# Attention, two gated products and a maximum of three in float32: scores a block ahead, and operands prepared at another place

## The chip, the cores and the metric

One core of one Trainium2 chip. The time is device microseconds of one launch. Before: 1257.44 us, median of three runs (1254.42 to 1262.59). The engines are TensorE (PE), VectorE (DVE), ScalarE (ACT), GpSimd (POOL) and SyncE (SP); each works its own instructions in order and waits on semaphores that the others raise. DMAs are started by SP and POOL.

## The reference

```python
# attention: 4 x 8 heads, 768 tokens, 64 wide; chunks of 32 tokens see 8 memory keys, 16 to the left, 8 to the right
scores = scale * (q_c @ k_full.T); scores -= max(scores)
a = exp(scores); a = a / (sum(a) + 1e-09)
x = a @ v_full                                   # then x: 3072 tokens x 512
h = x @ w_in                                     # 512 -> 2048
y = (h * cos(h)) @ w_out                         # 2048 -> 512
z = maximum(maximum(y @ w1, y @ w2), y @ w3)     # 512 -> 768
out = z @ w_out2                                 # 768 -> 512
```

Everything is float32.

## The kernel before

**Numbers.** A matmul on the fast float32 form rounds its operands, so each operand is held in two parts: `high`, a rounded copy that ACT makes, and `low`, the remainder that DVE (for w_in POOL) makes from raw and high. A product is three matmuls (`three`, L544 to L548): high x high, high x low, low x high. Of the four large products, the last three are done by seven products of half-size blocks in place of eight; for that, DVE or POOL first forms four sums of each raw operand (`sums_g`, `sums_w2`, `sums_h` and others, seven 256-column pieces per operand), then ACT rounds the seven pieces (1792 columns) and DVE makes the low part.

**First stage (L650).** Eight blocks `t` of 384 tokens. A block is 16 half tiles `f` of h (`hidden`, 12 matmuls of 384 columns each); two half tiles are a tile, which ACT evacuates (`evacuate`, two passes), DVE reduces to a turn (`turn`), ACT takes through Sin and Square (`cosine`) and DVE multiplies (`gated`); POOL stores it to DRAM. One tile later the same for the next, with two pairs of banks. Between the half tiles PE does the attention of the next block (`attend`, L615) for its three groups of 128 tokens: `scores_of`, after which DVE takes maximum and difference (`shift`) into the one probability buffer and ACT the exponential of all three (`exps`, L780); `turn_probs`, copied by ACT (`copy_probs`); `values`, scaled by DVE (`normalise`); `turn_out`, rounded by ACT and DVE into x (`x_high`, `x_low`). In blocks after the first the scores, the transposes, the weighted values and x's transposes have one bank each. q/k and v of the first three groups have a buffer each, later groups share one of each kind, and SP loads a group when PE is done with the one before. w_in is loaded by POOL through three buffers, converted in block 0.

**Second product (L673).** 48 units `n`, eight to a block `b` of 512 tokens; a unit is 42 matmuls of 256 columns. g's operand is loaded by SP (two raw buffers, `load_g`), summed by DVE, rounded by ACT (`high_g`), and its rest made by DVE (`low_g`, L1096), two units ahead, into three slots. At the last unit of a block ACT copies two of the seven sums out (y11 and p5, L938 and L943) and DVE adds the others; PE opens a bank again when it has been read. SP stores y at the next unit, ahead of that unit's load of g; the loads of y come in the same queue.

**Third stage (L764).** 36 units of the three products with maximum (384 columns; nine to a block, three weights times three), then 12 of the last product (256 columns, two to a group of 512 tokens). In each step ACT copies three sums out (`snap`), DVE adds and compares (`c22`, `c11`, `c12`, `c21`, `largest`). In the first block of this stage the weights are converted on the way: POOL loads w2's unit and forms sums (`load_w2`, `sums_w2`), ACT and DVE do high and low at the end of step `n` for unit `n + 1`. For the last product z comes back from DRAM: SP loads (`load_h`), DVE sums, ACT and DVE round, at the end of the step that the list `HIGH_H` (L67) names for each of the 18 operands `r`; two steps of PE wait for three of them. The last stores of z and the loads share SP's queue.

The waits that order all this are written out by hand; three of them at the heart of it:

```python
pe.wait_ge(shifted, n)                 # scores_of: the bank is read
dve.wait_ge(pt_done, n - NSUB + 1)     # shift: the probabilities of the block before are turned
act.wait_ge(unit_done, n - 2)          # high_g: the slot is free
```

## Time and profile before

| | |
|---|---|
| runs | 1262.59, 1254.42, 1257.44 us |
| profiled execution | 1261.36 us, span 1259.6 us |
| mean granted TensorE clock | 0.919 |
| PE busy | 1037.5 us, 82% of the span |
| DVE busy | 686.4 us, 54% |
| ACT busy | 512.6 us, 41% |
| POOL busy | 156.4 us, 12% |
| HBM traffic | 107 GB/s over the span |

The busy time of an engine is the sum of its instructions; the clock is the share of full speed that PE was granted. The span is cut, by what PE works on, at 36.9 us (first half tile of h), 93.0 (block 1), 447.5 (block 7), 481.0 (first unit of the second product), 818.6 (first step of the third stage) and 922.4 (second block of it); the last product begins near 1119 us.

### The profile page before, as it was taken

The page shows a single profiled execution, that of the slowest core. Times are in us where ns is not written, and L with a number is a line of the kernel's source. Part 1 is how long each engine was busy: PE and PEld are TensorE (multiplying, and loading weights), DVE is VectorE, ACT ScalarE, POOL GpSimd, SP SyncE. Part 2 cuts the span into 40 slices and gives each one's busy share as a digit, 9 for nine tenths or more (in the row PEclk, how much of TensorE's full clock was granted, in tenths as well). Part 3 has the DMA queues.
Part 4 walks back from the last instruction along what each step waited for, and adds up shares of the span by engine and source line. Part 5 has one row for each costly group of instructions (what it writes and reads, how often), then busy time and mean ns, then how long its engine had stood idle before and what let it go on. Part 6 is the DMA issues. An engine that isn't in the chain of part 4 may idle for free.

```text
span 1259.6 us, 18304 instructions
## 1 busy us (share of the span) xinstructions
PE 1037.5 (82%) x7564; PEld 997.0 (79%) x7564; DVE 686.4 (54%) x926; ACT 512.6 (41%) x641; POOL 156.4 (12%) x199
## 2 busy tenths in 40 slices
PE   5797877888788799688778686877699999996887
PEld 4687777777777799688778686777699999986876
DVE  4444545354535467656666565844464646675462
ACT  1575646556555686322323232323232323433231
POOL 3540101010101112100100000044110001100000
PEclk6998989899989999989898897989899999998888
DMA  9654445353534335232332324142111211233331
GB/s 200 170 150 125 139 115 145 106 160 106 153 109 135 92 112 165 84 117 87 113 103 84 101 84 151 37 133 74 59 76 51 75 45 49 92 118 101 117 101 67
DMA packets 73587, 135.41 MB, mean 108 GB/s; under 512 B 5920, under 2 KB 39712, under 8 KB 73504
## 3 DMA queue, kind: packets, MB, share of 16 engines
q1 hardware_dynamic: 61856, 94.39, 25.9%
q0 software_dynamic: 11648, 39.85, 9.4%
q8 instruction: 60, 0.98, 0.4%
q14 instruction: 23, 0.19, 0.1%
HBM read 87.03 MB, written 47.19 MB: 107 GB/s over the span
## 4 chain that ended last, share of the span: by engine, by line
PE 41%; DVE 25%; ACT 15%; DMA 11%; issue 6%; SPq 2%; DVEq 0%; ACTq 0%
PE ps L546 12%; PE ps L548 12%; PE ps L547 12%; DVE units L1099 7%; ACT units L831 5%; DMA work<-qk_in 4%; DMA work<-v_in 3%; DMA work<-g_dram 2%; PE ps L587 2%; PE ps L562 2%; DVE work L1088 2%; DVE work L1086 2%; DVE work L1090 2%; ACT work L808 1%; DVE units L1143 1%
## 5 line engine op out<-in xcount | busy, mean ns | idle before, releaser
L546 PE MATMUL ps<-units 128*128 128x384 f32 (+1 forms) x1940 | 644.1, 332 | 124.9 <-DVE units L1099 44.7
L547 PE MATMUL ps<-units 128*128 128x384 f32 (+1 forms) x1940 | 628.6, 324 | 0.0
L548 PE MATMUL ps<-units 128*128 128x384 f32 (+1 forms) x1940 | 627.9, 324 | 0.0
L546 PEld LDWEIGHTS ps<-units 128*128 128x128 f32 x1940 | 394.1, 203 | 144.7 <-issue 83.4
L547 PEld LDWEIGHTS ps<-units 128*128 128x128 f32 x1940 | 394.1, 203 | 0.0
L548 PEld LDWEIGHTS ps<-units 128*128 128x128 f32 x1940 | 393.0, 203 | 0.0
L831 ACT CAST units<-work 128x1792 fp32r<-128x1792 f32 x48 | 80.9, 1686 | 233.8 <-DVE work L1090 233.8
L965 ACT COPY work<-ps 128x384 f32<-128x384 f32 (+1 forms) x144 | 63.6, 453 | 221.3 <-PE ps L548 221.3
L1058 DVE SCALAR_TENSOR_TENSOR work<-work 128x768 f32<-128x768 f32 x64 | 62.7, 980 | 148.1 <-ACT work L808 148.1
L1099 DVE TENSOR_TENSOR units<-work,units 128x1792 fp32r<-128x1792 f32 x48 | 97.1, 2023 | 70.1 <-ACT units L831 70.1
L805 ACT ACTIVATE work<-ps 128x768 f32<-128x768 f32 x64 | 51.8, 809 | 130.9 <-PE ps L548 130.2
L441 POOL DMA_DIRECT2D g_dram<-work x64 | 46.5, 727 | 361.8 <-DVE work L1063 355.0
L1278 DVE TENSOR_TENSOR work<-work,ps 128x384 f32<-128x384 f32 (+1 forms) x48 | 24.9, 519 | 115.5 <-PE ps L548 115.5
L1063 DVE SCALAR_TENSOR_TENSOR work<-work 128x768 f32<-128x768 f32 x64 | 61.9, 968 | 42.0 <-ACT work L815 41.9
L808 ACT ACTIVATE work<-ps,rounder 128x768 f32<-128x768 f32 x64 | 57.3, 896 | 1.6 <-DVE work L1063 1.6
L815 ACT ACTIVATE work<-work 128x768 f32<-128x768 f32 x64 | 54.1, 845 | 2.0
L813 ACT ACTIVATE work<-work 128x768 f32<-128x768 f32 x64 | 54.0, 844 | 0.1
L562 PE MATMUL ps<-work 128*32 128x128 f32 x704 | 26.9, 298 | 32.8 <-DMA work<-qk_in 18.2
L562 PEld LDWEIGHTS ps<-work 128*32 128x32 f32 x704 | 20.4, 118 | 39.0 <-issue 38.9
L1143 DVE TENSOR_TENSOR units<-work,units 128x1792 fp32r<-128x1792 f32 x18 | 36.1, 2024 | 17.7 <-ACT units L871 17.5
L465 POOL DMA_DIRECT2D work<-w_in x12 | 6.5, 549 | 313.6 <-DVE units L1105 294.7
L1299 DVE TENSOR_TENSOR work<-work,ps 128x384 f32<-128x384 f32 (+1 forms) x48 | 24.9, 519 | 35.8 <-PE ps L548 35.7
(100 smaller groups left out, 806.5 us busy)
## 6 DMA issues: line engine op xcount, KB each, us to landing
g_dram<-work POOLq DMA_DIRECT2D x64, 384.0 KB, 3.6
work<-g_dram SPq DMA_DIRECT2D x48, 512.0 KB, 3.8
work<-qk_in SPq DMA_DIRECT2D x44, 384.0 KB, 5.3
work<-w_in POOLq DMA_DIRECT2D x50, 256.0 KB, 3.2
work<-v_in SPq DMA_DIRECT2D x44, 256.0 KB, 4.1
...
```

Source lines behind the costliest of these rows:

```text
L546: pe.matmul(o, wh, mh, start=start, stop=False, skip_group_check=onto)
L547: pe.matmul(o, wh, ml, start=False, stop=False, skip_group_check=onto)
L548: return pe.matmul(o, wl, mh, start=False, stop=stop, skip_group_check=onto)
L562: mm = pe.matmul(scores(n)[chunk, a, :, :], q[:, a, KC + CH * c:KC + CH * c + CH], two_parts(q, a, c, KC + SUB), start=True, stop=True)
L808: act.activation(ang(i), hidden_banks(i), ACT.Identity, scale=1.0 / (2 * PI), bias=rounder[:, :])\
L813: act.activation(ang(i), ang(i), ACT.Sin, scale=BELOW_PI).then_inc(sin_done, 1)
L815: act.activation(ang(i), ang(i), ACT.Square, scale=ROOT_TWO).then_inc(square_done, 1)
L831: act.copy(operand(9 + n % 3)[:, 0, :, :], graw[n % 2]).then_inc(g_high, 1)
L965: act.copy(tile[:, 0:span_of(n)], bank).then_inc(copied, 1)
L1058: dve.scalar_tensor_tensor(out=ang(i), in0=ang(i), scalar=ROUND, in1=hid(i), op0=ALU.subtract, op1=ALU.subtract).then_inc(r_done, 1)
L1063: dve.scalar_tensor_tensor(out=hid(i), in0=ang(i), scalar=1.0, in1=hid(i), op0=ALU.subtract, op1=ALU.mult).then_inc(g_done, 1)
L1099: dve.tensor_tensor(g[:, 1, :, :], graw[n % 2], g[:, 0, :, :].bitcast(F32), ALU.subtract).then_inc(g_ready, 1)
```

## The change

In the first stage the order of the attention's steps among the half tiles changes. Three buffers of q/k serve the groups up to the ninth and three of v those up to the sixth, where they served the first three, and v's loads are whole rows. In block `t` (from 1 on) PE turns the probabilities of block `t + 1` and does the scores of block `t + 2`, whose exponential ACT takes at half tile 14; block 0 does the scores of blocks 1 and 2. w_in gets 16 raw buffers in space that later operands use, and SP loads it. `high_g` and `low_g` work in two parts, four pieces and three, of which the first needs two of the four sums. ACT copies y11 before it rounds g. The first load of y moves from unit 40 to unit 24 in SP's queue, and the preparations of y and of w2 in the second product move. In the third stage weights and h are rounded at the head of a step, w2 for unit `n + 2`; a part of h's sums goes to POOL; `HIGH_H` names earlier steps for eight operands, and SP loads h by that list. The diff, cut:

```diff
-HIGH_H = (32, 33, 34, 35, 36, 37, 38, 38, 39, 40, 40, 41, 42, 42, 43, 44, 44, 45)
+HIGH_H = (32, 33, 34, 35, 36, 37, 37, 38, 38, 39, 40, 40, 41, 42, 42, 43, 44, 44)
...
+        raw_rows = [plain(f"raw_wi{i}", at, 512 * n) for i, (at, n) in
+                    enumerate(((2560, 2), (UCOLS + 2560, 2), (2 * UCOLS + 2048, 3), (3 * UCOLS + 2048, 3),
+                               (4 * UCOLS, 6)))]
+        raw_wi = [rows[:, 512 * i:512 * (i + 1)] for rows, n in zip(raw_rows, (2, 2, 3, 3, 6)) for i in range(n)]
...
+        def sums_h(eng, r):
+            done, base = h_sums[r % 3], 4 * (r // 3)
+            t = raw_d[r % 3]
+            eng.wait_ge(h_landed[r % 3], 16 * (r // 3) + 16)
...
             load_qk(0)
+            load_qk(1)
             load_v(0)
-            load_qk(1)
+            load_wi(0)
             load_qk(2)
             load_v(1)
             load_v(2)
-            load_qk(NSUB)
-            load_v(NSUB)
-            for n in range(NSUB + 1, SUBS, NSUB):
+            for f in range(1, 6):
+                load_wi(f)
+            for n in range(NSUB, 2 * NSUB):
                 load_qk(n)
-                load_qk(n + 1)
-                if n + 2 < SUBS:
-                    load_qk(n + 2)
+                load_wi(2 * n)
+                load_wi(2 * n + 1)
+            for n in range(NSUB, 2 * NSUB):
                 load_v(n)
-                load_v(n + 1)
-                if n + 2 < SUBS:
-                    load_v(n + 2)
+                if n < 2 * NSUB - 1:
+                    load_wi(2 * n + 6)
+                    load_wi(2 * n + 7)
+            for n in range(2 * NSUB, 3 * NSUB):
+                load_qk(n)
+            load_v(2 * NSUB)
+            load_qk(3 * NSUB)
+            for n in range(2 * NSUB + 1, SUBS):
+                load_v(n)
+                if n + 3 < SUBS:
+                    load_qk(n + 3)
             for n in range(4):
...
-                if n == UNITS1 - FPAIRS:
+                if n == 3 * FPAIRS:
                     load_y(0)
...
-                if m % TAUS == 0:
-                    for r in range(NPAIR * (m // TAUS + 2), min(NPAIR * (m // TAUS + 3), HUNITS)):
+                for r in range(2 * NPAIR, HUNITS):
+                    if max(HIGH_H[r - NPAIR], UNITS_A + 1) == UNITS_A + 1 + m:
                         load_h(r)
...
-            load_wi(0)
...
-            pool.wait_ge(v_landed[0], 32)
-            load_wi(1)
-            load_wi(2)
...
-                if f + 3 < NF:
-                    pool.wait_ge(wi_ready, f + 1)
-                    load_wi(f + 3)
...
+            for r in range(HUNITS):
+                if r < 2 * NPAIR or r % 2 == 0:
+                    sums_h(pool, r)
...
+            def attend_first(f):
+                n = NSUB
+                if f == 0:
+                    scores_of(n)
+                elif f == 2:
+                    scores_of(n + 1)
+                elif f == 4:
+                    scores_of(n + 2)
+                elif f == 7:
+                    turn_probs(n)
+                elif f == 9:
+                    values(n)
+                    turn_probs(n + 1)
+                elif f == 10:
+                    turn_out(n)
+                    turn_probs(n + 2)
+                elif f == 11:
+                    values(n + 1)
+                    scores_of(n + NSUB)
+                elif f == 12:
+                    turn_out(n + 1)
+                    scores_of(n + NSUB + 1)
+                elif f == 13:
+                    values(n + 2)
+                elif f == 14:
+                    turn_out(n + 2)
+                    scores_of(n + NSUB + 2)
...
                 n = NSUB * (t + 1)
-                if t < NBLK - 1:
...
+                later = t < NBLK - 2
+                if f == 1:
+                    turn_probs(n)
+                elif f == 3:
+                    values(n)
+                elif f == 4:
+                    turn_probs(n + 1)
+                    turn_out(n)
+                elif f == 6:
+                    turn_probs(n + 2)
+                    if later:
                         scores_of(n + NSUB)
+                elif f == 7:
+                    values(n + 1)
+                elif f == 8:
+                    turn_out(n + 1)
+                elif f == 9 and later:
+                    scores_of(n + NSUB + 1)
+                elif f == 11:
+                    values(n + 2)
+                elif f == 12:
+                    turn_out(n + 2)
+                    if later:
+                        scores_of(n + NSUB + 2)
...
+            scores_of(0)
+            scores_of(1)
+            turn_probs(0)
+            values(0)
+            scores_of(2)
...
-                    attend(t, f)
+                    if t == 0:
+                        attend_first(f)
+                    elif t < NBLK - 1:
+                        attend(t, f)
...
+            def high_g(n, part):
+                act.wait_ge(g_sums, 4 * n + 2 * part + 2)
+                if part == 0:
+                    if n < 3:
+                        act.wait_ge(h_done, TILES - FPAIRS + (2, 4, 5)[n])
+                    else:
+                        act.wait_ge(unit_done, n - 2)
+                q = slice(0, 4) if part == 0 else slice(4, 7)
+                act.copy(operand(9 + n % 3)[:, 0, q, :], graw[n % 2][:, q, :]).then_inc(g_high, 1)
...
+                if u == UNITS - 1:
+                    act.wait_ge(w2_ready, u)
                 raw = raw_late if u >= 3 and u % 2 else raw_w
                 act.copy(operand(s)[:, 0, :, :], raw).then_inc(w2_high, 1)
 
@@ -861,7 +937,7 @@
                 act.copy(operand(SLOT_V[v])[:, 0, :, :], raw_d[v]).then_inc(v2_high, 1)
 
             def high_h(r):
-                act.wait_ge(h_sums, 4 * r + 4)
+                act.wait_ge(h_sums[r % 3], 4 * (r // 3) + 4)
                 if r < 6:
                     act.wait_ge(p_done[4], UNITS_A - UNITS + 3 + r + 1)
                 elif r < 9:
...
+                    if first and f == 5:
+                        exps(0, NSUB, n + NSUB)
                     if f % 2:
                         i = FPAIRS * t + f // 2
                         evacuate(i)
+                        if first and f == 7:
+                            copy_probs(n)
+                        elif first and f == 9:
+                            copy_probs(n + 1)
+                        elif first and f == 15:
+                            exps(0, NSUB, n + 2 * NSUB)
+                        elif f == 1 and not last and not first:
+                            copy_probs(n)
...
+                    elif not last:
+                        if f == 4:
+                            copy_probs(n + 1)
+                            x_high(n)
+                        elif f == 6:
+                            copy_probs(n + 2)
+                        elif f == 8:
+                            x_high(n + 1)
+                        elif f == 12:
+                            x_high(n + 2)
+                        elif f == 14 and t < NBLK - 2:
+                            exps(0, NSUB, n + 2 * NSUB)
+                    if 1 <= t < 6 and f == 10:
                         high_w1(t - 1)
...
-                if n and n + 2 < UNITS1:
-                    high_g(n + 2)
                 if i == FPAIRS - 1:
                     act.wait_ge(whole_done[1], b + 1)
                     if b:
                         act.wait_ge(y_stored[(b - 1) % 2], y_total(b - 1))
                     act.copy(y11, ps[:, BANK1[1], :]).then_inc(y1_copied, 1)
+                if n and n + 2 < UNITS1:
+                    high_g(n + 2, 0)
+                    high_g(n + 2, 1)
+                if i == FPAIRS - 1:
...
                 if n == 41:
                     high_y(0, 1)
+                    high_y(0, 5)
                 elif n == 42:
-                    high_y(0, 5)
-                elif n == 43:
                     high_y(0, 2)
                     high_y(0, 6)
+                elif n == 43:
+                    high_y(0, 3)
+                    high_y(0, 7)
                 elif n == 44:
-                    high_y(0, 3)
+                    high_y(0, 4)
                 elif n == 45:
-                    high_y(0, 7)
-                    high_y(0, 4)
-                elif n == 46:
                     high_w2(1)
+                elif n == 47:
+                    high_w2(2)
...
+                if 1 <= n <= 6:
+                    high_w2(n + 2)
+                if UNITS_A - 7 <= n < UNITS_A - 4:
+                    high_v2(n - UNITS_A + 7)
+                rows = [r for r in range(HUNITS) if HIGH_H[r] == n]
+                if rows:
+                    high_h(rows[0])
                 if n < UNITS_ALL:
                     snap(n, 1, bank_b(n), snap1, c11_done, n, s1_copied)
                     if n < UNITS_A and u == UNITS - 1 and blk < NBLK2 - 1:
                         high_y(blk + 1, 1)
+                    if rows[1:]:
+                        high_h(rows[1])
...
-                if 1 <= n <= 7:
-                    high_w2(n + 1)
-                if UNITS_A - 7 <= n < UNITS_A - 4:
-                    high_v2(n - UNITS_A + 7)
-                for r in range(HUNITS):
-                    if HIGH_H[r] == n:
-                        high_h(r)
...
+            def low_g(n, part):
+                dve.wait_ge(g_high, 2 * n + part + 1)
+                q = slice(0, 4) if part == 0 else slice(4, 7)
                 g = operand(9 + n % 3)
-                dve.tensor_tensor(g[:, 1, :, :], graw[n % 2], g[:, 0, :, :].bitcast(F32), ALU.subtract).then_inc(g_ready, 1)
+                low = dve.tensor_tensor(g[:, 1, q, :], graw[n % 2][:, q, :], g[:, 0, q, :].bitcast(F32), ALU.subtract)
+                if part:
+                    low.then_inc(g_ready, 1)
...
+                        elif f == 8:
+                            sums(0, NSUB, NSUB + 1)
+                    elif f == 2 and not last:
+                        sums(0, NSUB, NSUB + t + 1)
...
+                    if first:
+                        if f == 9:
                             normalise(n)
                         elif f == 10:
+                            x_low(n)
+                        elif f == 11:
                             normalise(n + 1)
+                            shift(n + NSUB)
+                        elif f == 12:
+                            shift(n + NSUB + 1)
+                            x_low(n + 1)
+                        elif f == 13:
+                            normalise(n + 2)
+                        elif f == 14:
+                            shift(n + NSUB + 2)
+                            x_low(n + 2)
+                    elif not last:
+                        if f == 3:
+                            normalise(n)
+                        elif f == 4:
                             x_low(n)
+                        elif f == 6 and t < NBLK - 2:
+                            shift(n + NSUB)
+                        elif f == 7:
+                            normalise(n + 1)
+                        elif f == 8:
+                            x_low(n + 1)
+                        elif f == 9 and t < NBLK - 2:
+                            shift(n + NSUB + 1)
                         elif f == 11:
                             normalise(n + 2)
                         elif f == 12:
-                            x_low(n + 1)
-                        elif f == 13:
+                            if t < NBLK - 2:
+                                shift(n + NSUB + 2)
                             x_low(n + 2)
-                    if 1 <= t < 6 and f == 12:
+                    if 1 <= t < 6 and f == 5:
                         sums_w1(t - 1)
-                    if 1 <= t < 6 and f == 15:
+                    if 1 <= t < 6 and f == 14:
                         low_w1(t - 1)
...
                     low_w2(0)
-                if n == 41:
-                    y_sum(0, 0)
-                elif n == 42:
+                if n in (30, 31):
+                    y_sum(0, n - 30)
+                elif n == 41:
                     y_low(0, 1)
                     y_low(0, 5)
-                    y_sum(0, 1)
+                elif n == 42:
                     y_sum(0, 2)
-                elif n == 43:
                     y_low(0, 2)
                     y_low(0, 6)
+                elif n == 43:
                     y_sum(0, 3)
+                    y_low(0, 3)
+                    y_low(0, 7)
                 elif n == 44:
-                    y_low(0, 3)
+                    y_low(0, 4)
                 elif n == 45:
-                    y_low(0, 7)
-                    y_low(0, 4)
-                elif n == 46:
                     low_w2(1)
+                elif n == 47:
+                    low_w2(2)
...
+                rows = [r for r in range(HUNITS) if HIGH_H[r] == n]
+                if 1 <= n <= 6:
+                    low_w2(n + 2)
+                if UNITS_A - 7 <= n < UNITS_A - 4:
+                    v2_low(n - UNITS_A + 7)
+                if rows:
+                    low_h(rows[0])
                 if n:
                     c22(before)
                     if before < UNITS_A and before % NB2:
                         largest(before)
                 if renew:
                     y_low(blk + 1, 1)
+                if rows[1:]:
+                    low_h(rows[1])
                 if n < UNITS_ALL:
                     c11(n)
+                for r in range(2 * NPAIR, HUNITS):
+                    if r % 2 and HIGH_H[r] == n + 1:
+                        sums_h(dve, r)
...
```

## Rows read from the trace of the kernel before

**Rows 1.** windows: us, busy of PE, PEld, DVE, ACT, POOL, clock, DMA share, GB/s

```profile
36.90:93.00 56.10, 45.49 (x409) 42.13 (x410) 24.58 (x29) 36.91 (x51) 29.92 (x33) 0.97 0.61 167
93.00:447.50 354.50, 286.38 (x2417) 265.38 (x2417) 170.04 (x217) 203.32 (x251) 41.80 (x58) 0.92 0.45 128
447.50:481.00 33.50, 33.50 (x193) 33.50 (x194) 25.17 (x33) 28.98 (x35) 6.89 (x10) 1.00 0.34 117
481.00:818.60 337.60, 269.73 (x2018) 264.72 (x2017) 218.09 (x293) 100.43 (x76) 15.14 (x19) 0.91 0.32 100
560.00:584.00 24.00, 24.00 (x202) 24.00 (x201) 15.38 (x21) 7.91 (x5) 0.00 (x0) 1.00 0.33 103
818.60:922.40 103.80, 77.27 (x385) 74.90 (x384) 46.61 (x55) 29.61 (x44) 38.53 (x46) 0.90 0.24 81
922.40:1107.00 184.60, 184.01 (x1056) 182.80 (x1056) 106.34 (x148) 57.75 (x104) 10.18 (x12) 1.00 0.19 71
1107.00:1259.60 152.60, 119.36 (x828) 116.19 (x828) 80.53 (x128) 47.04 (x72) 0.00 (x0) 0.88 0.30 99
```

**Rows 2.** waits of PE: line, what it waited for, us in total, times, longest us

```profile
PE ps L546 <- DVE units L1099: 44.7, 15, 8.5
PE ps L573 <- ACT work L784: 28.1, 7, 4.0
PE ps L546 <- DVE units L1105: 26.0, 7, 4.8
PE ps L546 <- DVE units L1143: 24.7, 5, 5.0
PE ps L546 <- ACT work L938: 20.0, 5, 4.2
PE ps L587 <- DMA work<-v_in: 19.6, 9, 3.4
...
PE ps L546 <- ACT work L965: 4.9, 8, 1.1
```

**Rows 3.** timeline of PE around 606 us: start, us, line, shapes, idle before it

```profile
606.64 0.58 PE L546 MATMUL ps<-units 128*128 128x256 f32 x1 [4.83 <-DVE units L1099]
...
612.57 0.40 PE L546 MATMUL ps<-units 128*128 128x256 f32 x1
...
613.04 0.28 PE L546 MATMUL ps<-units 128*128 128x256 f32 x1
```

**Rows 4.** timeline of POOL, one load of w2 and its first sum

```profile
860.35 1.08 POOL L465 DMA_DIRECT2D work<-w_in  x2 [3.49 <-DVE units L1105]
864.04 0.73 POOL L474 TENSOR_TENSOR work<-work 128x256 f32<-128x256 f32 x1 [2.61 <-DMA work<-w_in]
```

**Rows 5.** timeline of PE, one group of scores

```profile
226.06 1.08 PE L562 MATMUL ps<-work 128*32 128x128 f32 x32 [1.96 <-DMA work<-qk_in]
```

**Rows 6.** timeline of ACT ahead of an Exp

```profile
172.12 0.81 ACT L805 ACTIVATE work<-ps 128x768 f32<-128x768 f32 x1 [6.15 <-PE ps L548]
...
174.49 0.84 ACT L815 ACTIVATE work<-work 128x768 f32<-128x768 f32 x1
175.35 1.28 ACT L784 ACT_TABLE_LOAD   x1
176.65 1.48 ACT L784 ACTIVATE work<-work 128x1536 f32<-128x1536 f32 x1
```

**Rows 7.** timeline of DVE, the gating of the same tile

```profile
175.37 0.96 DVE L1063 SCALAR_TENSOR_TENSOR work<-work 128x768 f32<-128x768 f32 x1 [0.58 <-ACT work L815]
```

**Rows 8.** timeline of DVE at a boundary of the second product

```profile
594.93 0.68 DVE L1246 TENSOR_TENSOR work<-work,ps 128x512 f32<-128x512 f32 x1
601.01 0.42 DVE L1084 TENSOR_TENSOR work<-work 128x256 f32<-128x256 f32 x1 [5.40 <-DMA work<-g_dram]
...
604.56 2.02 DVE L1099 TENSOR_TENSOR units<-work,units 128x1792 fp32r<-128x1792 f32 x1 [1.75 <-ACT units L831]
```

**Rows 9.** timeline of SP, first loads of h behind the last store

```profile
1129.26 4.96 SPq L352 DMA_DIRECT2D work<-h_dram  x2
```

221 lines of the change are left out of this document (94 added, 127 removed).

## Prediction

> **What bounds the kernel now.** First I cut the span where its stages change and read the busy times by window [rows 1]. TensorE (PE) is the engine with the most work, and two windows show what it does when nothing stops it: the last block of the first stage (447.50 to 481.00, no attention) is 33.5 us for 193 matmul records, all busy at clock 1.00, and 922.40 to 1107.00 is 184.0 us busy of 184.6. So a long dense stretch keeps the full clock here. Everything else is a loss against that: the six attention blocks take 354.5 us (59.1 each) at clock 0.92, the 48 units of the second product take 337.6 us at 0.91, the first nine steps of the third stage 103.8 us, the end 152.6 us at 0.88.
>
> Second, who PE waited for [rows 2]. The order is by total, but the count and the longest matter more: 4.0 us seven times for the Exp, some 4.9 us five times for h (L1143), up to 4.8 us seven times for w2 (L1105), 4 us five times for the y11 copy (L938), and L1099 with 44.7 us over 15. These are regular stalls of a schedule, not of a saturated engine.
>
> Third, what a stall costs beyond itself [rows 3]. After 4.83 us of idleness a 256-column matmul lasts 0.41 us in the place of 0.28; 28 of them stand 0.21 apart where full speed has 0.12, which is 2.7 us more: the lower of the two levels, 1.2 and 2.4 GHz. A stall of 4 to 5 us costs about 2.7 beyond its length; where the wait is 2 to 3 us I count half of that, as an estimate between nothing and 2.7.
>
> **Front (before the first hidden matmul, 36.9 us).** The loads of scores 1 go ahead of the values of 0, scores 2 go behind values 0, and w_in's loads leave POOL for SP. The first score groups wait on loads, the rest on a chain of ACT and DVE steps. Bounds: no gain (the same bytes must land) to 8 us (the load of one group taken out of the way twice, at the 3.7 us of the w2 load [rows 4]). I take 4, nearer the chain, which stays.
>
> **Block 0.** It loses the waits for q/k and v, for there are three buffers, but takes three more score groups of 1.08 us [rows 5] and both exponentials, and ACT also converts w_in. One exponential is a table load of 1.28 and 1.48 us of work [rows 6], and another table load leads back to Sin, so two cost ACT 8.1 us in a block where it is already busy 36.9 of 56.1 [rows 1]. I take no change, between 5 us gained and 5 lost.
>
> **Blocks 1 to 6.** Pure work is 33.5 + 3 score and 3 value groups of 1.08 + six groups of transposes at an estimated 0.4 (four 128-column matmuls, between 4 times 0.06 by the 256-column spacing and 1.08) = 42.4 us. What goes: the Exp wait, since it ran at half tile 14 of the block before; the score wait for the shift; and q/k and v loads, whose buffers are now freed three or four half tiles (2.09 us each) and their attention groups ahead, 8 us and more, against 6.2 us now (two half tiles and the wait of 1.96 [rows 5]). The v loads also go row by row in one piece. If that cover failed, v alone would bring back what [rows 2] shows for it, 19.6 us in all.
> What is late next is `turn_out`. It stands one half tile behind its `values`, and DVE does `normalise` only after `gated`, which waits for ACT. From the end of an odd half tile ACT takes 3.23 us for evacuation, Sin and Square [rows 6], `gated` 0.96 [rows 7], and `normalise` is like the 128x512 add of 0.68 [rows 8]: ready after 4.9 us. PE gets there after 1.08 + 2.09 = 3.2 us (3.6 with transposes between). That is 1.7 us, twice a block. At the first one ACT is behind: the Exp at half tile 14 makes 3.23 + 1.28 + 1.48 = 6.0 us for a slot of 4.2, the Sin reload adds 1.28, and each tile gives back about 1 us, so 1.3 us are left: 2.7 us. Together 6.1 us a block, and 1.5 us for a low stretch behind the first. A block is then 50.0 us, and block 6, without scores ahead, 46.8: 296.8 for six, 58 less. Bounds 35 (the waits double) to 72 (half of them hidden).
> The table load is the one place where a rule would move the sum. The row shows Square of 0.84 us beginning at 174.49, the load at 175.35 and Exp at 176.65 [rows 6]: a switch costs 1.3 us. The Trainium skill (ScalarE: Activation LUTs, What ACT_TABLE_LOAD costs) counts a drain of about 1.38 us beside the load, 2.66 us in all, for each switch. By it ACT would be 2.8 us later after each Exp and the sum about 17 us worse; the trace has no such drain, so I do not take it.
>
> **Second product, 48 units.** A unit is 42 matmuls; 202 in 24.00 us [rows 1] make it 4.99 us, 240 for 48, so 98 us are lost now. (a) The y11 copy stands before the rounding of g, where ACT is free once the first product has been summed; five waits of 4 us and their low stretches go. What is queued behind it is the rounding, 0.6 us later, with two units of slack. (b) In two parts the chain of one g is two sums 0.9, high part 4/7 of the 1.75 that DVE waits for it = 1.0, low parts 4/7 and 3/7 of 2.02 = 1.15 and 0.87, some 4.0 us, where now sums, rounding and remainder follow one another for 5.6 us (601.01 to 604.56 + 2.02) [rows 8]; 5.6 is over the unit's 4.99, 4.0 is not. (c) The store of y ahead of the next g load stays. From the last add of y (594.93) to the sums of g (601.01) are 6.1 us, and that add will begin 7.3 us after the start of its unit (two adds end at 2.9, the low parts at 4.9, then five adds 0.6 apart); the g is ready 17.4 us after it, PE wants it after 15.0: 2.4 us left of 4.8. (d) `load_y(0)` is moved, not removed: the longest wait on L1099, 8.5 against 4.8, puts its price at 3.7 us, now at unit 24. Left over: 4 x 2.4 + 6.1 = 15.7, about 5 for low stretches, 1 for w1 at the start and 3 for the y operands at the end: 265 us, 73 less (55 to 85).
>
> **Third stage, first nine steps.** 385 matmuls at 33.5/193 us are 66.8 us, so 37 are lost. Unit n + 1 was rounded behind step n; now n + 2 is, at the head, so the rounding itself is covered by a step of 42 x 0.174 = 7.3 us. Next is POOL: load to sums 3.7 us, four sums of 0.8 us [rows 4], 7.0 to 8 us a unit, about PE's pace. And ACT and DVE now wait at the head for those sums, with the copies of the step's sums queued behind them, for which PE's sixth and fourth products wait. w2 unit 2 is some 2.5 us late and unit 3, which may load only when the last unit is done, some 5 us; with the drift of POOL and one low stretch 13 us stay: 24 less (10 to 32).
>
> **End.** The waits on L1143 are 24.7 us, with about 2.7 each for the clock 38, and 5 on L965 [rows 2]: 43 lost. The sums of h on POOL, and rounding two steps earlier, cover 6.2 + 1.7 + 2 us of chain. But r = 6 is due at step 37, where its load leaves SP only behind the last store of the group before, 2.1 us into that step (1129.26) [rows 9]. It lands some 4.3 us later (3.7 for the smaller w2 load [rows 4]), four sums are 3.2, rounding 1.75: 11.4 us into the step, and the copy that PE's sixth product needs at 5.3 is queued behind it. That is 6 us, 2.7 for the clock and 2 of small waits: 11 stay, 32 less (20 to 40).
>
> **Sum.** 4 + 0 + 58 + 73 + 24 + 32 = 191 us. The profiled execution took 1261.4 us (span 1259.6 and 1.8 around it), 3.9 above the median of 1257.4; 1261.4 - 191 = 1070, and 1068 set between that and the same against the median.
>
> **Rivals.** *ACT becomes the bound of the blocks*: its copies, both table loads and the wait of `x_high` for `turn_out` add up, so a block keeps 59 us. For it: ACT has no gap between evacuation and Square [rows 6]; against: busy 203 of 354.5 us [rows 1]. 1068 + 58 = 1126, chance 0.14, in which I count that the scores are not really ahead because one probability buffer holds them.
> *The heads block*: ACT waits at the head of steps and stalls the copies, so fill and end win nothing: 1068 + 56 = 1124, chance 0.08.
> *g stays late*: only the y11 copy is won, 34 of 73 us: 1107, chance 0.08.
> *A table switch costs twice its row*: with ACT's queue full, the load of 1.28 is preceded by as long a pause. Two in each of six blocks are 2.6 us, all on the first wait: 16 us, 1084, chance 0.05. The rule of the Trainium skill named above (ScalarE: Activation LUTs, What ACT_TABLE_LOAD costs) says this.
> *Less is left*: `turn_out` finds its input because PE's pace gives ACT time: 6 x 7.6 us less, 1022; chance 0.13. That block 0 showed small waits at clock 0.97 speaks for it.
> *Slower*: the clock in the attention blocks. Three short waits a block could hold it at the low level throughout. A block's 42 us double, less the 6 of waits: 36 each, 216 for six, 1284. It decides from more than 5.3 of the six blocks at the low level. Against: the blocks now have longer waits and still 0.92 and 0.97 [rows 1]. Chance 0.02.
>
> **Numbers.** My forecast has 0.50. The range 1030 to 1128 takes the unknown terms' bounds, most of the rivals and half of *less is left*. A change of 1%, 13 us, is about what can be told from none. Faster by more than 1%: 0.96; within it 0.02 (several rivals at once); slower 0.02.
>
> **What would show it.** Blocks of 50 us with waits on the vector engine's L1045 line before `turn_out` and none on v, q/k or Exp; no wait on the y11 copy; one wait of 2 to 3 us each eight units; steps of 7.3 us in the fill but for the first two; one wait of 6 us at step 37. Wrong if blocks stay near 59 us, or if ACT's copies are what PE waits for in the third stage.

## The result, and the profile after

The kernel after takes 1103.65 us, the median of four runs (1098.38 to 1105.35), beside 1255.93 us of the kernel before, four runs: ratio 0.8775, interval 0.8726 to 0.8824. The profiled execution has a span of 1101.0 us, 158.6 less than before, at a mean granted clock of 0.957. The forecast was 1068 us, with a range of 1030 to 1128: the direction and the range held, and the point lies 36 us too low.

The same cuts as before, by what PE works on, give this table of windows (us, then busy of PE, PEld, DVE, ACT, POOL, then clock, DMA share, GB/s; PEld is TensorE's loading of weights). First the kernel before, cut on its very first matmuls, for the third stage up to the last product and for the last product, which [rows 1] does not have as one line:

```profile
818.40:1118.40 300.00, 272.07 (x1502) 268.39 (x1501) 162.10 (x214) 92.41 (x154) 48.71 (x58) 0.97 0.21 75
1118.40:1259.60 141.20, 108.78 (x769) 105.69 (x768) 71.58 (x117) 42.00 (x63) 0.00 (x0) 0.87 0.30 99
```

Then the kernel after: front, block 0, blocks 1 to 6, second product, third stage, last product. Block 7, left out here, takes 33.5 us as before.

```profile
0.00:33.20 33.20, 20.41 (x233) 16.31 (x233) 14.89 (x26) 7.96 (x14) 9.76 (x17) 0.63 0.99 215
33.20:99.60 66.40, 53.04 (x505) 47.70 (x506) 29.50 (x36) 36.45 (x51) 24.92 (x23) 0.90 0.73 175
99.60:409.20 309.60, 269.28 (x2351) 248.93 (x2351) 164.10 (x210) 204.58 (x251) 41.41 (x57) 0.97 0.48 137
...
442.70:720.90 278.20, 253.12 (x2018) 250.46 (x2017) 222.40 (x340) 105.37 (x123) 14.28 (x19) 0.96 0.39 123
720.90:994.80 273.90, 266.19 (x1502) 262.72 (x1502) 157.63 (x201) 93.00 (x155) 68.73 (x79) 0.99 0.24 83
994.80:1101.00 106.20, 95.51 (x770) 94.89 (x768) 58.17 (x81) 38.92 (x62) 31.34 (x28) 0.97 0.37 127
```

| part | before | after | change | predicted |
|---|---|---|---|---|
| front | 36.9 | 33.2 | -3.7 | -4 |
| block 0 | 56.1 | 66.4 | +10.3 | 0 (-5 to +5) |
| blocks 1 to 6 | 354.5 | 309.6 | -44.9 | -58 |
| second product | 337.5 | 278.2 | -59.3 | -73 |
| third stage, up to the last product | 300.0 | 273.9 | -26.1 | -24 |
| last product | 141.2 | 106.2 | -35.0 | -32 |

Part of block 0's 66.4 us is this one execution: in the seven other kernels that keep its order of steps (experiments 4 and 6 to 11) the block takes 62.6 to 64.4 us.

Busy time of the other engines barely tells of it (DVE 672.2 us for 686.4, ACT 515.6 for 512.6, POOL 197.7 for 156.4): what went are waits, and with them the low level of TensorE's clock. The waits of PE after, against [rows 2] (line, what it waited for, total, times, longest):

```profile
PE ps L629 <- DVE o_natural L1144: 47.0, 21, 6.9
PE ps L579 <- DVE units L1199: 22.5, 8, 8.2
PE ps L579 <- ACT work L1062: 13.7, 7, 6.4
PE ps L620 <- ACT prob_turned L862: 9.5, 10, 2.6
```

The Exp (28.1 us before), v (19.6), w2's rest (26.0), h's rest (24.7) and the copy of y11 (20.0) are gone from the list. What is new at its head is `turn_out` waiting for `normalise` (L1144), as the prediction said. A block has one wait of 3.1 us and two of 1.6 (timeline of PE, the waits in brackets):

```profile
116.57 0.66 PE L629 MATMUL ps<-ident,o_natural 128*128 128x128 f32 x4 [3.10 <-DVE o_natural L1144]
...
131.62 0.66 PE L629 MATMUL ps<-ident,o_natural 128*128 128x128 f32 x4 [1.59 <-DVE o_natural L1144]
...
144.68 0.66 PE L629 MATMUL ps<-ident,o_natural 128*128 128x128 f32 x4 [1.59 <-DVE o_natural L1144]
...
168.77 0.99 PE L629 MATMUL ps<-ident,o_natural 128*128 128x128 f32 x4 [3.10 <-DVE o_natural L1144]
```

From 116.57 to 168.77 is the period of a block: 52.2 us, before 59.1, predicted 50.0. DVE's timeline ahead of the first of them shows why the wait is there at all:

```profile
111.94 1.75 DVE L1129 TENSOR_REDUCE ssum<-work 128x24 f32<-128x1536 f32 x1
...
114.15 0.90 DVE L1157 SCALAR_TENSOR_TENSOR work<-work 128x768 f32<-128x768 f32 x1
114.97 0.95 DVE L1162 SCALAR_TENSOR_TENSOR work<-work 128x768 f32<-128x768 f32 x1
115.83 0.68 DVE L1144 TENSOR_TENSOR o_natural<-ps,sinv 128x512 f32<-128x512 f32 x1
```

The normalisation (L1144) needs 0.68 us and stands behind the turn (L1157) and the gating (L1162) of a tile of h, which need what ACT makes of that tile. In front of those, at the first of the three, the sum over the probabilities (L1129) takes another 1.75 us. Little of that sum is on the path: ACT's last pass for this gating (L887) ends at 114.56, and the gating begins at 114.97.

### The profile page after: what moved, and what is told of

It reads as the page before. It is cut to its first block, busy times and chain, and to the rows that moved or that the text cites. A ratio compares the mean times of both kernels' runs of the same rounds, so it can differ in the third digit from the quotient of the medians.

```text
span 1101.0 us, 18400 instructions
## 1 busy us (share of the span) xinstructions
PE 991.0 (90%) x7564; PEld 954.5 (87%) x7564; DVE 672.2 (61%) x926; ACT 515.6 (47%) x689; POOL 197.7 (18%) x231
## 4 chain that ended last, share of the span: by engine, by line
PE 49%; DVE 16%; ACT 16%; DMA 10%; issue 5%; POOL 3%; SPq 1%; DVEq 0%; ACTq 0%
PE ps L579 15%; PE ps L581 15%; PE ps L580 15%; DVE units L1199 5%; DMA work<-g_dram 3%; ACT work L885 3%; ACT work L887 2%; ACT work L880 2%; ACT work L877 2%; DVE work L1162 2%; PE ps L595 2%; ACT units L905 2%; PE ps L629 2%; DMA work<-w_in 1%; DMA work<-h_dram 1%
## 5 line engine op out<-in xcount | busy, mean ns | idle before, releaser
L579 PE MATMUL ps<-units 128*128 128x384 f32 (+1 forms) x1940 | 622.2, 321 | 41.6 <-DVE units L1199 22.5
L580 PE MATMUL ps<-units 128*128 128x384 f32 (+1 forms) x1940 | 612.0, 315 | 0.0
L581 PE MATMUL ps<-units 128*128 128x384 f32 (+1 forms) x1940 | 611.9, 315 | 0.0
L579 PEld LDWEIGHTS ps<-units 128*128 128x128 f32 x1940 | 378.0, 195 | 57.0 <-DVE units L1199 24.5
L580 PEld LDWEIGHTS ps<-units 128*128 128x128 f32 x1940 | 377.9, 195 | 0.0
L581 PEld LDWEIGHTS ps<-units 128*128 128x128 f32 x1940 | 377.4, 195 | 0.0
L905 ACT CAST units<-work 128x1024 fp32r<-128x1024 f32 x96 | 85.7, 938 | 154.8 <-DVE work L1185 141.7
L1062 ACT COPY work<-ps 128x384 f32<-128x384 f32 (+1 forms) x144 | 63.0, 453 | 136.9 <-PE ps L581 136.8
L1157 DVE SCALAR_TENSOR_TENSOR work<-work 128x768 f32<-128x768 f32 x64 | 61.9, 967 | 99.1 <-ACT work L880 99.1
L1199 DVE TENSOR_TENSOR units<-work,units 128x1024 fp32r<-128x1024 f32 x96 | 102.1, 1105 | 10.2 <-ACT units L905 10.2
L1162 DVE SCALAR_TENSOR_TENSOR work<-work 128x768 f32<-128x768 f32 x64 | 61.3, 957 | 47.8 <-ACT work L887 47.7
L629 PE MATMUL ps<-ident,o_natural 128*128 128x128 f32 x96 | 18.7, 329 | 47.0 <-DVE o_natural L1144 47.0
L629 PEld LDWEIGHTS ps<-ident,o_natural 128*128 128x128 f32 x96 | 12.0, 161 | 54.1 <-DVE o_natural L1144 53.3
L1234 DVE TENSOR_TENSOR units<-work,units 128x1792 fp32r<-128x1792 f32 x18 | 39.6, 2201 | 31.1 <-ACT units L947 31.1
L1400 DVE TENSOR_TENSOR work<-work,ps 128x384 f32<-128x384 f32 (+1 forms) x48 | 24.8, 516 | 55.3 <-PE ps L581 55.3
L887 ACT ACTIVATE work<-work 128x768 f32<-128x768 f32 x64 | 54.1, 846 | 2.0
L1183 DVE TENSOR_TENSOR work<-work 128x256 f32<-128x256 f32 x48 | 20.1, 420 | 35.7 <-DMA work<-g_dram 35.7
```

The costliest lines, as they stand in the source:

```text
L579: pe.matmul(o, wh, mh, start=start, stop=False, skip_group_check=onto)
L580: pe.matmul(o, wh, ml, start=False, stop=False, skip_group_check=onto)
L581: return pe.matmul(o, wl, mh, start=False, stop=stop, skip_group_check=onto)
L887: act.activation(ang(i), ang(i), ACT.Square, scale=ROOT_TWO).then_inc(square_done, 1)
L905: act.copy(operand(9 + n % 3)[:, 0, q, :], graw[n % 2][:, q, :]).then_inc(g_high, 1)
L1062: act.copy(tile[:, 0:span_of(n)], bank).then_inc(copied, 1)
```

## The experiments

"Before" and "after" are the two kernels. Where the stages of an experiment matter, they are cut at the same first matmuls as above. One fact is needed to read them: kernels with the same first stage begin their second product anywhere from 437.2 to 442.8 us (after itself 442.75, the HIGH_H experiment 437.22), so an effect in block 0 is read from its own waits and length and not from the total.

### 1. The copy of y11 ahead of the rounding of g, alone, on the kernel before

```diff
-                if n and n + 2 < UNITS1:
-                    high_g(n + 2)
                 if i == FPAIRS - 1:
                     ...
                     act.copy(y11, ps[:, BANK1[1], :]).then_inc(y1_copied, 1)
+                if n and n + 2 < UNITS1:
+                    high_g(n + 2)
```

> The kernel before, with one edit: at the last unit of a block of the second product ACT copies y11 ahead of the rounding of g. Theory: the copy is behind the rounding in ACT's queue and nothing else holds it, so the five waits of 4 us on it (20.0 us in all) and the low clock stretches behind them (5 times 1.6 us) go: 28 us less for the second product, 337.5 to 310 us, 1228 us in all. Rival: g is late anyway (its chain is 5.6 us a unit), so the waits turn up on the low part of g at the same units or the next, and less than 10 us is won.

Measured: 1245.72 us, ratio 0.9893 (0.9857 to 0.9930), 13 us less. The second product goes from 337.5 to 327.5 us. The waits on the copy are gone, but PE then waits for the additions to y, and for g as before:

```profile
527.48 0.38 PE L546 MATMUL ps<-units 128*128 128x256 f32 x1 [1.34 <-DVE work L1229]
...
544.89 0.58 PE L546 MATMUL ps<-units 128*128 128x256 f32 x1 [5.10 <-DVE units L1100]
```

So the 20 us of [rows 2] on L938, with their low stretches, were worth 10: the rest moved to the next link.

### 2. g rounded in two parts, alone, on the kernel before

```diff
-                act.copy(operand(9 + n % 3)[:, 0, :, :], graw[n % 2]).then_inc(g_high, 1)
+                for part, q in ((0, slice(0, 4)), (1, slice(4, 7))):
+                    act.wait_ge(g_sums, 4 * n + 2 * part + 2)
+                    ...
+                    act.copy(operand(9 + n % 3)[:, 0, q, :], graw[n % 2][:, q, :]).then_inc(g_high, 1)
```

(and so for the remainder, `low_g` on DVE.)

> The kernel before, with one edit: rounding and remainder of g in two parts of four and three pieces, the order of the queues as before. Theory: the chain of one g falls from 5.6 to 4.0 us and the waits on g at units 3 to 7 (7.8 us) go; the five at the block's third unit lose 1.5 us each, but the y11 copy still waits behind both parts: 16 us less, 1240 us in all. Rival: the copy of y11 comes 0.1 us later and the added instructions eat the rest: no change within 5 us.

Measured: 1201.03 us, ratio 0.9548 (0.9512 to 0.9584), 57.6 us less. The second product takes 282.3 us, 55 of the 59 that the whole change wins there. The line for the waits on g, 44.7 us in 15 of [rows 2], becomes

```profile
PE ps L546 <- DVE units L1102: 22.6, 8, 7.1
```

and of the five waits on the y11 copy one of 1.90 us is left, though the copy still stands behind the rounding. That is the point: ACT was late with the copy because it stood waiting for the sums of a late g. ACT's timeline in the kernel before shows it, with the copy (L938) at the end:

```profile
581.45 1.69 ACT L831 CAST units<-work 128x1792 fp32r<-128x1792 f32 x1 [3.81 <-DVE work L1090]
586.94 1.68 ACT L831 CAST units<-work 128x1792 fp32r<-128x1792 f32 x1 [3.81 <-DVE work L1090]
588.53 0.58 ACT L938 COPY work<-ps 128x512 f32<-128x512 f32 x1
```

The roundings are 5.49 us apart, and PE takes 5.04 us for a unit without a wait, so g falls behind by 0.45 us a unit. With two parts they follow every 4.00 us (535.16, 539.16, 543.16 in this experiment) until ACT has to wait for PE.

### 3. Both, on the kernel before

The edits of 1 and 2 together.

> The kernel before, with both edits of the second product: y11 copied first, g in two parts; the first load of y at unit 40 as before. Theory: the two add up to 28 + 16 and a little more, since after the copy the adds of y end sooner: 48 us less, 1208 us in all, with one wait of 2 to 3 us left in each block and 6 to 8 us at unit 42. Rival: they cover the same waits and together give no more than the larger one alone, 28 us.

Measured: 1196.33 us, ratio 0.9513 (0.9465 to 0.9561), 62 us less; second product 278.6 us, which is the 278.2 of after. The two edits are the whole gain of that stage, and the split carries it; alone 13 and 58, together 62: in part they remove the same stall.

### 4. w2 rounded one unit ahead at the end of a step again, on the kernel after

```diff
-                if 1 <= n <= 6:
-                    high_w2(n + 2)
 ...
+                if 1 <= n <= 7:
+                    high_w2(n + 1)
```

(the same for `low_w2` on DVE.)

> The changed kernel with one part taken back: w2 rounded at the end of step n for unit n + 1, unit 2 at the end of step 1, as before. Theory: the part was worth what the third stage lost of its waits (26 us between the two traces, of which h has next to nothing), so this kernel is 22 to 28 us slower than the changed one: 1129 us, with the seven waits of 2.7 to 4.8 us on w2's low part back. Rival: the earlier conversion of unit 1 and of y in the second product, which stays, already carries most of it: under 10 us slower.

Measured: 1128.09 us, ratio 0.8961 (0.8922 to 0.9001), 24.4 us more than after. The third stage takes 301.6 us, as before the change (300.0), and the seven old waits are back:

```profile
PE ps L579 <- DVE units L1205: 25.5, 7, 4.6
```

The gain of the third stage is this one move, in which the lead of a unit and the place at the head of a step were not tried apart. The time rises by less than the 27.7 us of the stage, since this execution reached its second product 3.9 us earlier than after.

### 5. `normalise` ahead of turn and gating, on the kernel after

```diff
+                    if not last and f in ((9, 11, 13) if first else (3, 7, 11)):
+                        normalise(n + ((9, 11, 13) if first else (3, 7, 11)).index(f))
                     if f % 2:
                         ...
-                        if f == 3:
-                            normalise(n)
```

(and so for the other five places.)

> The changed kernel with one edit: at the half tiles where DVE scales the weighted values it does so ahead of the turn and the gating, not behind them. Theory: the waits of 3.1, 1.6 and 1.6 us a block ahead of the transposes of the output (47.0 us over all blocks) are this order alone, since the values are there 1.1 us after the half tile and DVE is idle then; they go with the low clock stretch behind the first, 1.7 us a block: 55 us less, 1049 us. Rival: ACT, which rounds the turned output behind its own queue, is the bound, and the wait moves to x or to the next transposes: under 20 us less.

Measured: 1054.31 us, ratio 0.8398 (0.8354 to 0.8441), 49 us less than after. One wait of 1.6 us a block is left, and the block's period is 45.5 us:

```profile
195.94 0.66 PE L629 MATMUL ps<-ident,o_natural 128*128 128x128 f32 x4 [1.60 <-DVE o_natural L1144]
241.48 0.66 PE L629 MATMUL ps<-ident,o_natural 128*128 128x128 f32 x4 [1.60 <-DVE o_natural L1144]
```

A window over nearly four of these periods has clock 1.00:

```profile
147.90:329.00 181.10, 172.72 (x1621) 160.82 (x1622) 112.22 (x147) 134.99 (x165) 28.33 (x39) 1.00 0.59 162
```

6.3 us of waits a block in after, 1.6 here; 6.7 us of period less. The other 2 us are the low stretch behind the wait of 3.1. It also gives the work of PE in a block: 45.5 - 1.6 = 43.9 us, a wait of 0.3 on `copy_probs` included, where the prediction had 42.4.

Blocks 1 to 6 give 38 of the 49 us. Block 0 gives 9, or 6 against the 63.3 us that it takes in most other executions of this order:

```profile
30.89:87.98 57.09, 50.48 (x504) 45.84 (x505) 29.93 (x36) 36.35 (x50) 25.02 (x23) 0.94 0.83 205
```

That is 1.1 us more than the 56.0 of the kernel before, and the wait at the first `turn_out` is 1.82 us, for 6.91. Yet the stores of g still take 8.1 us to land here, and ACT still waits for one of them before it evacuates:

```profile
65.41 0.81 ACT L877 ACTIVATE work<-ps 128x768 f32<-128x768 f32 x1 [3.63 <-DMA g_dram<-work]
```

Experiments 6 and 11 ask about those stores; this one shows that most of block 0's loss is the order on DVE.

### 6. q/k of groups 7 and 8 loaded behind v of group 6, on the kernel after

```diff
-            for n in range(2 * NSUB, 3 * NSUB):
-                load_qk(n)
+            load_qk(2 * NSUB)
             load_v(2 * NSUB)
+            load_qk(2 * NSUB + 1)
+            load_qk(2 * NSUB + 2)
```

> The changed kernel with one edit in SP's queue: the loads of q/k for groups 7 and 8 stand behind that of v for group 6, so they leave some 15 us later in block 0. Theory: block 0 is 10 us longer than before because the 16 DMA engines are full until 72 us and the stores of the gated tiles take 8.1 us in the place of 3.6, for which ACT waits before it evacuates; with less in flight the stores land in 4 to 5 us, the wait of 6.9 us shrinks by 3 to 4 us and the kernel is 4 us faster, 1100 us. Rival: ACT's own work in block 0 (w_in, two Exp) makes that wait, and nothing changes within 1.5 us in block 0.

Measured: 1102.70 us, ratio 0.8779 (0.8736 to 0.8822), 1 us less than after, which is nothing that these runs can tell. The first wait of block 0 at `turn_out` falls all the same, from 6.91 to 3.48 us; in the five kernels with this part of the queue unchanged (experiments 4, 7, 8, 9 and 10) it is 5.2 to 6.2. The wait got shorter and the time did not: block 0 takes 63.1 us. Experiment 11 goes on from there.

### 7. The load of g ahead of the store of y, on the kernel after

```diff
+                if n >= 2 and n + 2 < UNITS1:
+                    load_g(n + 2)
                 if n % FPAIRS == 0 and n:
                     store_y(n // FPAIRS - 1)
                 if n == 3 * FPAIRS:
                     load_y(0)
-                if n >= 2 and n + 2 < UNITS1:
-                    load_g(n + 2)
```

> The changed kernel with one edit in SP's queue: in the second product the load of g goes ahead of the store of y (and of the load of y) of the same unit. Theory: the wait left at the third unit of each block (3.8, 2.4, 8.2, 2.8 and 2.3 us) is the load queued behind the store, which waits for the last add of y; all five go with their low stretches of 1.8 us: 26 us less, 1077 us. Rival: SP's wait on g's buffer then delays the store, and with it the next block's sums or the load of y, or g is late through DVE: under 8 us less.

Measured: 1073.76 us, ratio 0.8564 (0.8505 to 0.8623), 30 us less than after. The second product takes 252.2 us (278.2); it also began 3.8 us earlier, where nothing was edited. In after SP's queue at unit 24 reads, and DVE's sums begin 10 us late:

```profile
581.28 3.30 SPq L343 DMA_DIRECT2D y_dram<-work  x6
584.74 1.23 SPq L357 DMA_DIRECT2D work<-y_dram  x2
586.07 16.37 SPq L334 DMA_DIRECT2D work<-g_dram  x4
```

```profile
593.91 0.42 DVE L1183 TENSOR_TENSOR work<-work 128x256 f32<-128x256 f32 x1 [10.26 <-DMA work<-g_dram]
```

The line of waits on g, 22.5 us in 8, becomes

```profile
PE ps L579 <- DVE units L1199: 4.7, 5, 2.2
```

### 8. The list HIGH_H of the kernel before, on the kernel after

```diff
-HIGH_H = (32, 33, 34, 35, 36, 37, 37, 38, 38, 39, 40, 40, 41, 42, 42, 43, 44, 44)
+HIGH_H = (32, 33, 34, 35, 36, 37, 38, 38, 39, 40, 40, 41, 42, 42, 43, 44, 44, 45)
```

> The changed kernel with the list of steps for h as before (r = 6 at step 38 and seven others one step later), still at the head of a step and with sums on POOL. Theory: the wait of 6.4 us at step 37 is r = 6, whose load leaves 2 us into that step; a step later it is there, and the three operands that a pair of steps needs are rounded at the head of the step before: 7 us less, 1097 us. Rival: the last of the three is now rounded at the head of the step just before its use, so PE waits 1 to 3 us at each of five pairs: 5 us slower or no change.

Measured: 1095.14 us, ratio 0.8717 (0.8677 to 0.8757), 8.5 us less than after. The last product takes 99.1 us in the place of 106.2, which is the 7 us expected. The other 1.5 are scatter: without an edit there, the first stage of this execution was 5.5 us shorter than that of after, and the second product 3.6 us longer. The wait that goes is this one of after, on PE and, 2 us earlier, on ACT:

```profile
1014.22 0.58 PE L579 MATMUL ps<-units 128*128 128x256 f32 x1 [6.37 <-ACT work L1062]
```

```profile
1012.21 1.69 ACT L947 CAST units<-work 128x1792 fp32r<-128x1792 f32 x1 [7.70 <-POOL work L294]
1013.80 0.64 ACT L1062 COPY work<-ps 128x256 f32<-128x256 f32 x2
```

ACT stands 7.70 us for the sums of an operand that PE needs only later, with the copies that PE needs now queued behind it. So the earlier list costs. The rest of the change there carries the gain of the end, 141.2 to 99.1 us: rounding at the head of a step, sums on POOL, and SP's loads of h in the order of the list. No run tells these three apart.

### 9. The first load of y at unit 40 again, on the kernel after

```diff
-                if n == 3 * FPAIRS:
+                if n == UNITS1 - FPAIRS:
                     load_y(0)
```

(with its two sums moved from units 30 and 31 to 41 and 42.)

> The kernel after with the first load of y back at unit 40, in front of that unit's load of g, and its sums at units 41 and 42. My theory (the load's price is moved, not removed): the wait of PE on L1199 at unit 26, 8.2 us, falls to the 2.3 us of the other third units, one of some 6 to 8 us appears at unit 42, and the time stays within 4 us of the kernel after (1100 to 1108). Rival 1 (at unit 40 the load costs nothing, since little else is in the queue): some 8 us less, 1096. Rival 2 (late y also delays the sums and the first operands of the third stage): 6 us more or over, 1110.

Measured: 1100.88 us, ratio 0.8747 (0.8717 to 0.8777), 2.8 us less than after, within the 4 of the theory. The wait of 8.21 us at unit 26 is 3.21 now, and a new one stands at unit 42:

```profile
589.05 0.39 PE L579 MATMUL ps<-units 128*128 128x256 f32 x1 [3.21 <-DVE units L1199]
...
682.21 0.58 PE L579 MATMUL ps<-units 128*128 128x256 f32 x1 [6.20 <-DVE units L1199]
```

The load's price was moved, not removed.

### 10. Relu in the place of the exponential, on the kernel after

```diff
-                act.activation(p, p, ACT.Exp, scale=SCALE).then_inc(exp_done, 1)
+                act.activation(p, p, ACT.Relu, scale=SCALE).then_inc(exp_done, 1)
```

> The kernel after with Relu in the place of the exponential, so that the probabilities are not the reference's; it leaves out the exponential and with it both table loads of each block. My theory (the first wait of a block at turn_out, 3.1 us, is longer than the other two by ACT's lag behind the exponential and the return to Sin): it falls to the 1.6 us of the other two, its low stretch goes, and a block takes some 49 in place of 52 us: 15 to 20 us less over six blocks and block 0, 1085 to 1090. Rival (the first wait is set by the order of DVE alone and ACT's lag is covered): the wait stays at 3.1 us and the time within 4 us of the kernel after.

Measured: 1076.99 us, ratio 0.8563 (0.8532 to 0.8594), 26.7 us less than after. ACT has 14 instructions less, the table loads, and 18.9 us less busy time; the pass itself stays. The first wait of a block falls below the other two, and the period from one to the next is 48.3 us:

```profile
156.72 0.66 PE L629 MATMUL ps<-ident,o_natural 128*128 128x128 f32 x4 [1.15 <-DVE o_natural L1144]
170.16 0.66 PE L629 MATMUL ps<-ident,o_natural 128*128 128x128 f32 x4 [1.59 <-DVE o_natural L1144]
...
205.05 0.66 PE L629 MATMUL ps<-ident,o_natural 128*128 128x128 f32 x4 [1.15 <-DVE o_natural L1144]
```

So what makes the first wait longer than the other two is ACT's lag from the two table loads around the exponential: 2 x 1.28 = 2.6 us less on ACT, 1.95 us less of wait, and 3.9 us less of period, since the low stretch behind it goes too. The rival is refuted. The gain was larger than the 15 to 20 us expected: 23.4 us of it are in blocks 1 to 6, six times 3.9.

### 11. Half of w_in's loads left out, on the kernel after

```diff
             def load_wi(f):
+                if f >= 8:
+                    return
 ...
-                act.wait_ge(wi_landed[f], 16)
-                act.copy(w_in(f)[:, 0, :, :], raw_wi[f]...)
+                act.wait_ge(wi_landed[f % 8], 16)
+                act.copy(w_in(f)[:, 0, :, :], raw_wi[f % 8]...)
```

> The kernel after without the second half of the loads of w_in: half tiles 8 to 15 are rounded from the raw data of 0 to 7, so h is not the reference's in its second half; the instructions of all engines stay. That takes 8 loads of 256 KB, 2.1 MB, out of the 9.0 MB that move from 33 to 72 us, 9 us at the 231 GB/s of that stretch. Block 0 takes 66.4 us in the kernel after, with a wait of 6.9 us at the first turn_out and one of 2.6 before the first values. My theory (block 0 is long because full DMA engines hold back the stores of g, for which ACT's evacuation waits): the stores land in 4 to 6 us in the place of 8.1, the wait of 6.9 falls to 2 to 4, block 0 takes 57 to 61 us, and the time falls by 5 to 10 us, to 1094 to 1099. Rival (ACT's own work, 36 us with both exponentials and the conversion of w_in, sets it, or the scattered loads of q/k and v, which stay): the waits stay within 1 us and block 0 at 65 us or more, the time within 2 us of the kernel after.

Measured: 1100.74 us, ratio 0.8749 (0.8724 to 0.8773), 2.9 us less than after. The mechanism is as expected. From 33 to 72 us, the issues with size and median us to landing, first of after, then without the loads:

```profile
q1 hardware_dynamic: 4321, 7.83, 94.8%
...
g_dram<-work POOLq DMA_DIRECT2D x3, 384.0 KB, 8.1
```

```profile
q1 hardware_dynamic: 3096, 5.64, 67.2%
...
g_dram<-work POOLq DMA_DIRECT2D x4, 384.0 KB, 3.6
```

ACT in after waits for such a store before it may evacuate:

```profile
69.80 0.81 ACT L877 ACTIVATE work<-ps 128x768 f32<-128x768 f32 x1 [2.94 <-DMA g_dram<-work]
```

Without the loads that wait is gone, and PE's at `turn_out` is 3.50 us, for 6.91 in after and 5.7 to 6.2 in experiments 4, 7, 8 and 9, which have all loads. The time is not as I expected. From the first half tile to the third `turn_out` it is 59.5 us; in those four experiments 59.4 to 60.6, and in after 62.4. The 3 us of after are at the very beginning of block 0. First after, then this kernel:

```profile
33.20:41.20 8.00, 8.00 (x55) 7.09 (x56) 1.39 (x2) 2.33 (x5) 7.28 (x6) 0.62 1.09 206
...
31.40:39.40 8.00, 7.85 (x72) 7.11 (x76) 1.94 (x3) 4.71 (x9) 7.43 (x7) 1.00 1.10 217
```

After begins at the low level (0.62 over 8 us, 55 matmuls for 72); in the nine other kernels built on after the clock is 1.00 there. Where the shorter wait went shows beside experiment 8, in a stretch from 24 us behind the first half tile to the third `turn_out`. First experiment 8, then this kernel:

```profile
56.47:91.96 35.49, 23.81 (x248) 21.07 (x247) 19.60 (x22) 18.46 (x27) 12.22 (x13) 0.86 0.57 155
...
55.40:90.90 35.50, 26.48 (x249) 23.33 (x247) 19.55 (x22) 18.58 (x27) 12.25 (x13) 0.81 0.37 109
```

Both take 35.5 us for the same matmuls. PE waits 2.7 us less here and is busy 2.7 us longer at a lower clock: this kernel has a low stretch from 82.4 to 85.4 us (0.60), as experiment 6 has one from 82.6 to 85.6 (0.69), where experiment 8 has 1.00. I read that as the wait given back as low clock; what decides when the level falls was not tried.

### 12. The best of these together

`normalise` first (5), g before y (7), the old list (8) and q/k later (6).

> The kernel after with four edits at once: normalise ahead of turn and gated, the load of g ahead of the store of y, the list HIGH_H of the kernel before, and q/k of groups 7 and 8 loaded behind v of group 6. Alone they measured 49, 30, 8.5 and 1 us less than the kernel after. Theory (they lie in different stretches and add up): 1103.7 - 49 - 30 - 8.5 - 1 = 1015, ratio 0.807 to 0.811. Rival (the blocks run faster, so that queues and engines that were covered come late: less than 70 of the 88 us are won): 1032 or more.

Measured: 1020.91 us, median of six (1019.91 to 1023.97), ratio 0.8121 (0.8097 to 0.8145): 83 us less than after, 236 less than the kernel before, taken beside it. That is 6 us above the 1015 expected. The windows are blocks 0 to 7, second product, last product; the third stage takes 273.9 us, as in after:

```profile
30.12:391.51 361.39, 341.76 (x3048) 320.13 (x3049) 218.84 (x281) 270.57 (x337) 73.67 (x90) 0.99 0.59 162
391.51:645.40 253.89, 246.79 (x2017) 245.15 (x2017) 222.36 (x340) 105.35 (x123) 14.39 (x19) 0.99 0.42 135
...
919.30:1018.10 98.80, 93.75 (x770) 92.94 (x768) 59.41 (x81) 39.14 (x62) 32.31 (x28) 1.00 0.40 137
```

The parts add up: against after -51.2 up to the second product, -24.3, 0 and -7.4 are the 82.9 us of the span. The 6 us short of the sum of the single experiments are of the size of the first stage's scatter, for experiments 7 and 8 alone began their second product 4 and 5.5 us earlier than after without an edit there. Nothing covered before came late. PE is busy 95% of the span.

## Why the prediction was right, and where it was not

**Front, third stage, last product: right in size, and in part shown in reason.** -3.7, -26.1 and -35.0 for -4, -24 and -32. The front is open: no experiment changed it alone, and it scatters (34.4 to 37.6 us in the four kernels with the old first stage, 30.1 to 33.2 in the ten with the new). Experiment 4 shows that the third stage's gain is w2 rounded two units ahead at the head of a step. The cost foreseen there, ACT at the head of a step with the copies behind it, is in the trace as 3.15 and 2.17 us on L1062 in the first two steps. The wait of 6 us at step 37 came as 6.37, and experiment 8 shows that it hangs on the list.

**Blocks 1 to 6: right in mechanism, 13 us too good.** The step that failed is the sum of pure work. The waits are 3.10 + 1.59 + 1.59 = 6.3 us for 6.1, and their places are the three foreseen. PE's work is 43.9 us a block (experiment 5) where I had 42.4: a group of scores or values occupies PE for 1.01 to 1.02 us, and four transposes for 0.35 to 0.6, but matmuls of another shape also start some 0.1 us after the last, and a small wait on `copy_probs` (0.31 at 161.87) was not in the sum. The low stretch was taken at 1.5 and comes out at 2.0. With 0.2 on the waits that is 2.2 us in each of six blocks. Experiment 10 confirms that the first wait has ACT's lag in it. DVE's sum of probabilities in front of the turn (L1129, 1.75 us) was left out of the chain and stands in it, though it delays the gating by only about 0.4 us.

**The table switch.** I took 1.28 us for a switch and no drain. In after the final Square of a tile begins at 50.81 and a cast at 51.56, the load at 52.70 directly behind it, and the way back is as tight:

```profile
56.41 0.89 ACT L880 ACTIVATE work<-ps,rounder 128x768 f32<-128x768 f32 x1
57.32 1.28 ACT L885 ACT_TABLE_LOAD   x1
58.61 0.85 ACT L885 ACTIVATE work<-work 128x768 f32<-128x768 f32 x1
```

In experiment 10 the 14 loads took 18.9 us of ACT's busy time with them, 1.35 each, and the wait fell by 1.95 us where two switches of 1.28 went. The Trainium skill (ScalarE: Activation LUTs, What ACT_TABLE_LOAD costs) counts 2.66 us with the drain for a switch. By it, as an estimate, the first wait would have been the predicted 2.7 and two drains of 1.38 more, 5.5 us; it is 3.1. The trace does not agree, and the measurement decides.

**Block 0: wrong by 7 to 10 us.** The step that failed is "I take no change, between 5 us gained and 5 lost". It named three more score groups of 1.08 us and did not add them, and it left out the term that it worked out for blocks 1 to 6: `turn_out` waiting for `normalise` behind turn and gating. That order stands in block 0 too, with waits of 6.91, 0.71 and 1.59 us. Experiment 5 turns it round: the three waits become one of 1.82 us, and the block takes 57.1 us, 6.2 less than the 63.3 of most executions and 1.1 more than before. Some 3 us more of the 66.4 are the low clock at the beginning of that one execution. The full DMA engines, which I suspected first, are a link that exists: from 33 to 72 us the stores of g land in 8.1 us and not in the 3.5 of before, and ACT's evacuation waits for them. But experiments 6 and 11 shorten the wait that hangs on it and not the block, and in experiment 5 the block is short with the stores as late as ever.

**Second product: right in direction, wrong in whom to thank, 14 us too good.** The step "(a) five waits of 4 us and their low stretches go" credited the place of the copy; alone it wins 10 us of that stage, the two parts of g alone 55 (experiments 1 and 2). The argument in (b), a chain of 5.6 us for a unit of 4.99, was the right one and should have been carried through (in the trace 5.49 for 5.04): a chain longer than the unit makes everything behind it late, the copy too. The sizes: (c) and (d) are waits of 3.81, 2.40, 8.21, 2.77 and 2.28 us, 19.5 where I had 15.7; experiments 7 and 9 show that they hang on SP's queue. The low stretches behind these five are 9.2 us and not 5: I counted half a stretch for a wait of 2 to 3 us, and the two units after such a wait lose 1.74 us. The other waits make 5.5 where I had 4, a unit is 5.04 us and not 4.99, 2 us in all, and 2 us more are spread thinly.

**The rivals.** *ACT becomes the bound* did not come: a block takes 52.2 us and not 59. *The heads block* did not either: its waits are 6.4 us at the end and 3.2 and 2.2 in the fill, and both stages won what was forecast. *g stays late*: of the 44.7 us on g's rest 22.5 stay, those behind SP's queue, but the stage won 59 us where this rival gave 34. *Less is left* did not come of itself; experiment 5 is that case made by hand, and 38 of its 49 us lie in blocks 1 to 6, for which the rival had 46. *Slower*: the waits of 1.6 us leave no low stretch behind them (clock 1.00 in experiment 5). That the total came out as near as it did has some luck in it: the copy of y11 was credited with more than it won and the parts of g with less, within one stage.
